# Attention, gated feed-forward and token mixing on one core: two load tables, the order of loads on SP, and the place of one drain and one table load on ScalarE

## The reference, cut to what matters

```
attention: q, k, v of (4 batches, 8 heads, 576 tokens, 64)
  scores = q k^T / 8, masked; heads 0-3: the last 32 tokens; heads 4-7: every 4th of the last 128
  x = softmax(scores) v, as (4, 576, 512)
feed-forward: xk, xr = mixes of x and x shifted by one token (mu_k, mu_r)
  x = sigmoid(xr w_r) * (relu(xk w_k)^2 w_v)
token mixing: u = x + (tokens mixed by U V);  out = u + relu(u w_ch1) w_ch2
```

## Time and profile before

| | |
|---|---|
| median of 3 runs | 749.31 us (749.15 to 749.69) |
| the profiled execution, its own time | 749.15 us |
| its span, first to last instruction | 747.4 us |
| TensorE busy | 728.1 us, 97% |
| VectorE, ScalarE, GpSimd busy | 327.8, 301.4, 164.9 us |
| granted TensorE clock | 1.000, full speed |

### The profile page before, as it was taken

The page is one execution under the profiler, slowest core; times in us unless marked ns, Lnnn a source line. Parts: engine busy times, 40 slices in busy tenths (PEclk is TensorE's granted clock), DMA queues, the critical chain, the costliest instruction groups (busy, mean ns, idle before and its releaser), DMA issues.

```text
span 747.4 us, 13078 instructions
## 1 busy us (share of the span) xinstructions
PE 728.1 (97%) x4852; PEld 635.4 (85%) x4852; DVE 327.8 (44%) x687; ACT 301.4 (40%) x813; POOL 164.9 (22%) x253
## 2 busy tenths in 40 slices
PE   4899999999999999999999999999999999999998
PEld 3668888888888887888898999998899898999997
DVE  5888886688677536624322221312221131213111
ACT  3778777777767666644331111111111111111110
POOL 6699220202212151435860000000000000000000
PEclk9999999999999999999999999999999999999999
DMA  7994556455433410002440102101010210111001
GB/s 136 211 210 77 119 116 130 93 129 104 107 81 93 120 57 1 30 28 88 139 121 5 43 1 43 42 0 32 11 42 0 42 42 0 20 22 43 0 1 42
DMA packets 165458, 48.98 MB, mean 66 GB/s; under 512 B 142496, under 2 KB 159392, under 8 KB 165408
## 3 DMA queue, kind: packets, MB, share of 16 engines
q1 hardware_dynamic: 128704, 43.99, 23.7%
q10 hardware_dynamic: 36704, 4.34, 3.8%
HBM read 34.98 MB, written 9.37 MB: 59 GB/s over the span
## 4 chain that ended last, share of the span: by engine, by line
PE 91%; DVE 3%; ACT 2%; DMA 1%; issue 1%; ACTq 1%; SPq 1%; POOL 1%; DVEq 0%
PE bank L1411 28%; PE bank L1413 28%; PE bank L1412 28%; PE bank L1469 3%; PE bank L1432 2%; PE bank L1569 1%; ACTq L854 1%; ACT probs L844 1%; PE bank L1581 1%; POOL w_l L734 1%; PE bank L1452 0%; PE bank L1516 0%; DVE probs L1163 0%; DMA stage<-in_moe_w_ch_dram 0%; PE bank L1445 0%
## 5 line engine op out<-in xcount | busy, mean ns | idle before, releaser
L1378 DVE SCALAR_TENSOR_TENSOR h_l<-bank,h_h 128x384 fp32r<-128x384 f32 x96 | 53.5, 558 | 289.8 <-ACT h_h L1100 289.7
L1100 ACT ACTIVATE h_h<-bank 128x384 fp32r<-128x384 f32 x96 | 47.2, 491 | 317.8 <-PE bank L1413 317.8
L1413 PE MATMUL bank<-ut_h,w_l 128*128 128x384 f32 x384 | 129.4, 337 | 0.0
L1411 PE MATMUL bank<-ut_h,w_h 128*128 128x384 f32 x384 | 129.3, 337 | 0.0
L1412 PE MATMUL bank<-ut_l,w_h 128*128 128x384 f32 x384 | 128.9, 336 | 0.0
L1413 PE MATMUL bank<-w_h,h_l 128*128 128x512 f32 x288 | 113.7, 395 | 0.0
L1412 PE MATMUL bank<-w_l,h_h 128*128 128x512 f32 x288 | 113.5, 394 | 0.0
L1411 PE MATMUL bank<-w_h,h_h 128*128 128x512 f32 x288 | 112.0, 389 | 0.0
L1411 PE MATMUL bank<-xs_h,wk_h 128*128 128x256 f32 x288 | 83.6, 290 | 1.0 <-ACT sig L985 0.7
L1412 PE MATMUL bank<-xs_l,wk_h 128*128 128x256 f32 x288 | 81.0, 281 | 0.0
L1413 PE MATMUL bank<-xs_h,wk_l 128*128 128x256 f32 x288 | 80.9, 281 | 0.0
(11 more groups left out here) (124 smaller groups left out, 1151.2 us busy)
## 6 DMA issues: line engine op xcount, KB each, us to landing
stage<-in_moe_w_ch_dram SPq DMA_DIRECT2D x16, 512.0 KB, 3.3
out_dram<-result SPq DMA_DIRECT2D x18, 256.0 KB, 2.0
u_tile<-result SPq DMA_DIRECT2D x80, 48.0 KB, 2.0
probs_dram<-probs_blocks SPq DMA_DIRECT2D x12, 240.0 KB, 2.2
probs_t<-probs_dram SPq DMA_DIRECT2D x36, 80.0 KB, 2.2
k_raw<-in_k_dram ACTq DMA_DIRECT2D x64, 40.0 KB, 2.3
q_raw<-in_q_dram SPq DMA_DIRECT2D x64, 40.0 KB, 2.2
q_raw<-in_q_dram SPq DMA_DIRECT2D x64, 32.0 KB, 2.1
```

Of the source, the lines that this page charges most:

```text
L1100: act.activation(h_h[:, m % KRING, :], h_bank[m % 2][:, 0:C2], ACT.Relu).then_inc(hh_done, 1)
L1378: dve.scalar_tensor_tensor(h_l[:, m % KRING, :], h_bank[m % 2][:, 0:C2], 0.0, h_h[:, m % KRING, :].bitcast(F32), op0=ALU.max, op1=ALU.subt ...
L1411: pe.matmul(dst, lhs[0], rhs[0], start=start, stop=False)
L1413: return pe.matmul(dst, lhs[1], rhs[0], start=False, stop=stop)
```

## The change

ScalarE drains C(1,2) in slot 5 like every other step, that is behind the sigmoid of r1 and no longer behind that of r0. The dummy exponential and the key loads of (2,3) stand at the end of unit 5 and no longer of unit 6.

On SP the queries of (k+1, 3) come one slot earlier, and the values of (k+1, 0) two slots later, for the pairs that these tables govern. Of the query loads only those with p = 1 stay between the out issue and the back issues of a slot; those with p = 2 and p = 3 are issued behind the back issues and the values of the slot, as those with p = 0 already were. As a list for slots 10 to 20 (Q queries, V values, out and back as above):

```diff
-Q_BEHIND = [4, 1, 3, 4]
-V_BEHIND = [1, 2, 3, 1]
+Q_BEHIND = [4, 1, 3, 3]
+V_BEHIND = [1, 4, 3, 1]
...
                 for n in behind("A", slot, RAWS, Q_BEHIND):
-                    if n % PAIRS:
+                    if n % PAIRS == 1:
                         load_qk(*divmod(n, PAIRS))
                 for k, p in pairs_in("T", slot):
                     probs_from_dram(k, p)
...
                 for n in behind("A", slot, RAWS, Q_BEHIND):
-                    if n % PAIRS == 0:
+                    if n % PAIRS != 1:
                         load_qk(*divmod(n, PAIRS))
...
                 for step in steps_in(slot):
-                    if step != ("C", 1, 2):
-                        attention(*step)
+                    attention(*step)
...
-                    if (c, n) == (0, UNIT["r", 0]):
-                        attention("C", 1, 2)
...
                             attention_slot(c * NUNIT + n)
-                            if (c, n) == (0, UNIT["r", T1 - 1] + 1):
+                            if (c, n) == (0, UNIT["r", T1 - 1]):
                                 act.activation(unused[:, :], zeros[:, :], ACT.Exp)
                                 load_keys(2, 3)
```

## The result

The changed kernel takes 753.56 us (median of 5, 752.42 to 755.06), the kernel before 749.31 us (749.15 to 749.89). The ratio is 1.0055, interval 1.0042 to 1.0068: 0.55% or 4.1 us slower. The forecast was 751.5 us with a range up to 753.0.

The account below looks back on a forecast made before the run. TensorE, busy 728.1 of 747.4 us, bounds the kernel, so only added or removed idle time counts. 749.15 + 2.0 (stretch to D(3,2), swallowing ScalarE's 0.2) + 0.4 (D(5,2)) = 751.55, said as 751.5 us; range 748.9 to 753.0.

Parts of the forecast that it names:

- ScalarE: Near 51-61 us: TensorE 0.64 us late at transposes C(1,3), 1.0 at scores B(2,1), 0.2 left after an existing 0.82 us wait.
- Rival 4: ScalarE's table load: a 1.38 us drain exists, hidden from the trace, delaying everything behind it; 752.9 us, chance 0.03.
- D(3,0): Output products of (3,0): TensorE waits 1.0 us (0.2 to 2.0) for values issued later by SP.
- D(3,1): Output products of (3,1): returned probabilities land at 109.5, when TensorE arrives already late; nothing more added.
- D(3,2): Output products of (3,2): out (3,2) issued at 111.8 behind queries (4,2) and (4,3); 2.0 us late in all.
- D(5,2): Output products of (5,2): last probabilities land near 183.5 against a start at 183.09; 0.4 us late (0 to 1.7).
- D(7,2) and the even k: Later chunks: at k+1 = 7 over a microsecond is left over; for even k+1 two value transfers of 1.2 us fit.
- The stretch costs what its last date costs, 2.0 us: SP's full queue for k+1 = 3: waits aren't added, ScalarE's 0.2 us is absorbed; 2.0 us in all (0.7 to 3.6).
- Rival 1: SP's queue has more room, dates at D(3,2) and D(5,2) just met; about 749.3 us (748.9 to 750.2), chance 0.26.
- Rival 3: Backlog grows: waits at D(3,0), D(3,2), D(5,0), D(5,2) at upper bounds, ScalarE's 1.0 added; 755.4 at most, case 753.2, chance 0.10.
- Rival 2: Faster: probability round trips get free of surrounding traffic, 0.2 and 0.6 us waits go; about 748.4 us (747.5 to 748.9), chance 0.09.
- the lower bound of the stretch: SP's stretch for k+1 = 3: 0.7 us if the chain's three landings take 1.8 us, taking off 1.3 or so.

## Why the prediction was off, point by point

The direction held, and so did the mechanism in SP's queue; its size didn't, and the fall of the clock was missing. 751.5 us was said, 753.56 was measured.

- *ScalarE.* Forecast: TensorE 0.64 us late at C(1,3), 1.0 us at B(2,1), 0.2 us behind C(2,0). Measured, by the starts counted from unit 6: 0.60 (2.11 us behind it against 1.51), 1.10 (5.25 against 4.15) and 0.12 (10.68 against 10.56). Right, and alone the edits are inside the interval of no change. No drain stands ahead of the table load in the new place either: the table load starts at 52.88, as the activation before it, the drain of C(1,2), ends at 52.87. Rival 4, and with it the figure of 1.38 us in the Trainium skill ("ScalarE: Activation LUTs", What ACT_TABLE_LOAD costs), isn't seen here:

```profile
52.18 0.69 ACT L834 ACTIVATE probs_t<-bank 96x640 f32<-96x640 f32 x1
...
52.88 1.28 ACT L996 ACT_TABLE_LOAD   x1
```

- *D(3,0).* Forecast 1.0 us, measured 1.04 (1.03 to 1.59 in the other runs with these values loaded late). Right, with some luck: the last transfer was to be issued at 98.5 and was at 99.63 (99.0 without the 0.6 us of the late start), since the one before it held SP for 1.1 us; but it landed after 1.8 us and not 2.4.
- *D(3,1).* Forecast nothing more: right, except for 0.44 us in one run.
- *D(3,2).* This is the step that failed first: "Out (3,2), at 108.25 now, is issued at 111.8 [...] So it is late by 2.0 us in all." It was issued at 113.68, and D(3,2) started 3.7 us later than before, 3.1 us without the 0.6 us that this execution was late from the start. What was too short: the landing of out(3,1), 2.8 instead of 2.4 us; and the eight query transfers, 4.97 us instead of 4.0, because one of them held SP for 1.5 us. The term "queries (4,2) and (4,3), 2.0 us each as that of 92.00" took the length of an undisturbed load, while the trace before has Q(4,3) itself at 2.8 us (2.7 in three other profiles with it in this place):

```profile
108.64 2.81 SPq L533 DMA_DIRECT2D q_raw<-in_q_dram  x4
```

The sum with 3.1 in place of 2.0 would have been 752.65.
- *D(5,2).* Forecast 0.4 us, measured a wait of 0.50 (0.38 to 0.88 in the other runs with at least a part of the changed order there). The number is right, the cause not shown: out(5,2) did go right behind eight query transfers, as forecast (181.70, these end at 181.60), but with the ScalarE edits alone the wait is 0.55, behind an out(5,2) that took 4.2 us to land.
- *D(7,2) and the even k.* No waits in this profile, as forecast. But "the same arithmetic leaves over a microsecond" for D(7,2) doesn't hold in general: 0.91, 0.65 and 0.33 us in three of the seven profiles with the whole or a part of SP's new order there, none in those with the order as before.
- *What was not in the sum.* "The stretch costs what its last date costs, 2.0 us" was wrong in kind as well: behind this wait the clock is at half for a while, which costs 1.5 us more. Of 14 executions of the changed kernel timed with the result, ten have a mean clock of 0.997 or 0.998 over the span; their median is 754.1 us. The four with 1.00 have 752.6 us. The difference of 1.5 us is the cost of the drop as the starts of the steps have it, and 752.6 is about what the waits alone make. The two sets overlap, since landings and issues scatter as well: two of the ten took 752.4 and 752.6 us, and the middle one of the five behind the median, 753.56, has a clock of 1.00. So the clock doesn't account for the median by itself. The range had no term for it, and the term for the waits was 1.1 us too small; the median fell 0.6 us outside.
- *Rivals.* Rival 1 (749.3) is about what remains when the stretch around part 3 is left as before: 1.0007, 749.8 us on this scale. Rival 3 came nearest to the time, with 753.2, but by adding waits at their bounds and without the clock; it isn't what happened. Rival 2: the waits of 0.2 and 0.6 us, at D(2,3) and D(5,3), are gone, but they are in other profiles with SP's order as before too, so this isn't shown to be its effect; D(3,0) and D(3,2) cost several times as much.
- *Slips in the working.* Three landings at 1.8 us take off 1.6 us and not 1.3, so the lower bound of the stretch is 0.4 us and not 0.7, and two thirds of rival 3 give 753.3. Neither moves the forecast.

What stays open: why the same wait is followed by a drop in one execution and not in another (2.18 us with and without), and why single landings take 4 us.

## What to carry to other kernels

A queue that issues transfers is a resource with its own timeline: look for stretches in which each issue begins as the last one ends, and read a moved load as work put into that stretch and taken out of another. Small loads issued inside a round trip that the queue must wait for anyway cost nothing here; the same loads behind it do, and two moves that cost little alone (0.0014 and 0.0007) cost more than their sum in one full stretch. Take the length of a load from its own row, with its long issues in, and not from an undisturbed one. On an engine that is busy throughout, cost a new wait as its length, and ask what the clock did behind waits of such a length in a run: here 1.5 us could come on top of a wait of 1.6 to 2.2 us.

## What the runs showed of the hardware that I had not expected

A single wait of TensorE, in a kernel that otherwise keeps it busy, can halve its clock. Over the profiles here, behind 51 us: the waits of 1.03, 1.04 (twice), 1.09 (twice), 1.11, 1.30, 1.38 and 1.39 us had no drop behind them, nor had the shorter ones. Those of 1.59, 1.64 (twice), 1.74, 2.07 and 2.18 us had one. One of 2.18 us and one of 1.99 us (at D(3,2) in the kernel with SP's new order up to slot 20) had none. Each of the six drops made the way to the next step 1.4 to 1.5 us longer, whatever the wait before it.

The waits before 51 us (5.6 to 6.0 us and some of about 2 us in every profile) are left out. The table of stretches gives 1.00 there, but in the changed kernel the products of one shape (lines 1408 to 1410, 128x256) begin 0.21 us apart up to 28.3 us and 0.12 us apart from 28.9 us on, so for this part the column doesn't tell at what speed TensorE ran.
